# A three-stage kernel on one core: the scaling of k moved from GpSimd to VectorE, with the order around it

## The reference

```python
# 1: retention (attention with a fixed decay)
scores = q @ k.T / sqrt(D)                       # (4, 8, 576, 576)
gamma = 1 - 2.0 ** (-5 - arange(H))
Dmat = where(i >= j, gamma ** (i - j), 0)
x = (scores * Dmat) @ v                          # tokens x 512
# 2: mixture of experts: two of eight per token
noisy = x @ w_gate + log1p(exp(x @ w_noise)) * noise
two largest of noisy, softmax over the two
out[token] += weight * (relu(x[token] @ w1[e]) @ w2[e])   # 512 -> 1024 -> 512
# 3
h = out @ w_in                                   # 512 -> 2048
y = (h * cos(h)) @ w_out                         # 2048 -> 512
```

## Time and profile before

| | us |
|---|---|
| median of 3 runs | 1010.4 (1009.32 to 1011.52) |
| the profiled execution | 1012.63 |
| its span, first to last instruction | 1010.7 |

### The profile page before, as it was taken

One profiled execution on the slowest core, in us unless ns is written; L12 is line 12 of the kernel. 1 busy time (PEld: TensorE's weight loads), 2 busy tenths in 40 slices (PEclk: granted clock), 3 DMA queues, 4 the chain that ended last, 5 costly groups with the idle time before them and its releaser, 6 DMA issues.

```text
span 1010.7 us, 17316 instructions
## 1 busy us (share of the span) xinstructions
PE 982.1 (97%) x6116; PEld 887.9 (88%) x6116; DVE 482.3 (48%) x928; ACT 426.0 (42%) x779; POOL 118.2 (12%) x122
## 2 busy tenths in 40 slices
PE   8989799999999999999999989999999999999997
PEld 7878689899898989989899989999999999999996
DVE  3685464434333333333333466555555555555554
ACT  1442434333333333333334465455555555555554
POOL 4375520000000000000000131101000001010000
PEclk9996899999999999999999999999999999999999
DMA  9985552525445172544524452101010011011000
GB/s 364 308 304 208 194 202 84 197 96 177 156 129 203 62 257 75 185 147 145 187 74 148 159 192 95 42 32 42 21 52 21 21 52 37 36 34 29 31 0 32
DMA packets 64359, 122.02 MB, mean 121 GB/s; under 512 B 5696, under 2 KB 31552, under 8 KB 64320
## 3 DMA queue, kind: packets, MB, share of 16 engines
q1 hardware_dynamic: 58080, 101.05, 29.4%
q0 software_dynamic: 6240, 20.45, 6.1%
HBM read 83.73 MB, written 37.75 MB: 120 GB/s over the span
## 4 chain that ended last, share of the span: by engine, by line
PE 86%; DVE 4%; DMA 4%; issue 2%; SPq 1%; ACT 1%; another core or an unknown queue 1%; ACTq 0%; DVEq 0%
PE ps L1448 20%; PE ps L1467 20%; PE ps L1284 15%; PE ps L1302 14%; PE ps L1322 3%; PE ps L1334 3%; PE ps L1397 2%; PE ps L1409 2%; PE ps L1270 2%; DMA gath<-x_slots 2%; PE ps L1209 1%; PE ps L1240 1%; PE ps L1217 1%; DMA y_slots<-y_sb 1%; PE ps L1194 1%
## 5 line engine op out<-in xcount | busy, mean ns | idle before, releaser
L1284 PE MATMUL ps<-xs,w_hi 128*128 (+1 forms) x784 | 182.9, 312 | 0.0
L1020 DVE TENSOR_TENSOR w_lo<-raw,w_hi 128x1024 fp32r<-128x1024 f32 x48 | 58.8, 1225 | 170.0 <-ACT w_hi L665 170.0
L1284 PEld LDWEIGHTS ps<-xs,w_hi 128*128 128x128 f32 x784 | 133.1, 188 | 0.8
L1448 PE MATMUL ps<-x_hi,w_hi 128*128 (+1 forms) x384 | 130.8, 341 | 0.1
L1448 PE MATMUL ps<-x_hi,w_lo 128*128 (+1 forms) x384 | 129.1, 336 | 0.0
L1448 PE MATMUL ps<-x_lo,w_hi 128*128 (+1 forms) x384 | 129.1, 336 | 0.0
L790 ACT ACTIVATE turns<-ps 128x384 f32<-128x384 f32 x96 | 47.2, 491 | 183.7 <-PE ps L1448 183.6
L1284 PE MATMUL ps<-xs,w_lo 128*128 (+1 forms) x392 | 121.2, 309 | 0.0
L1144 DVE TENSOR_SCALAR turns<-turns 128x384 f32<-128x384 f32 x96 | 37.3, 388 | 167.6 <-ACT turns L790 167.6
L1467 PE MATMUL ps<-w_hi,g_hi 128*128 128x512 f32 x288 | 112.6, 391 | 2.1 <-DVE g_lo L1155 2.1
L1467 PE MATMUL ps<-w_hi,g_lo 128*128 128x512 f32 x288 | 113.3, 393 | 0.0
(11 more groups left out here) (169 smaller groups left out, 1674.9 us busy)
## 6 DMA issues: line engine op xcount, KB each, us to landing
raw<-weights SPq DMA_DIRECT2D x80, 512.0 KB
y_slots<-zeros_sb SPq DMA_DIRECT2D x42, 256.0 KB, 3.7
gath<-x_slots SPq DMA_DIRECT2D x40, 256.0 KB, 3.5
y_slots<-y_sb SPq DMA_DIRECT2D x40, 256.0 KB, 2.1
qk<-qk SPq DMA_DIRECT2D x18, 512.0 KB
kv<-kv SPq DMA_DIRECT2D x18, 512.0 KB, 6.2
out<-out_sb SPq DMA_DIRECT2D x18, 256.0 KB, 2.1
x_slots<-zeros_sb SPq DMA_DIRECT2D x8, 256.0 KB, 8.2
```

The lines of the kernel that those rows point to most:

```text
L1020: tt(w_lo[:, at], raw[:, f % 2, :], w_hi[:, at].bitcast(F32), ALU.subtract).then_inc(split_done, 1)
L1284: last_one = nc.tensor.matmul(ps[5 + half][:, 0:HALF], w[:, at:at + P], xs[:, bass.ds(g % 2, 1), a, k, half * HALF:(half + 1) * HALF].rear ...
L1448: last_one = nc.tensor.matmul(h_bank(f)[:, 0:TB], w[:, cols], a[:, bass.ds(par, 1), k, :].rearrange("p a s -> p (a s)"), start=k == 0 and ...
```

## The change

The scaling of k leaves GpSimd's loop and becomes `decay_k` in VectorE's. VectorE's order becomes: scale, carry, decay_k, then second choice, sums, places, first choice, split. Counts and places of the first three groups are in the same steps (8, 12, 16), the counts behind the k_dec products; that of the fourth group is issued in step 18 behind the rows. The eight zero tails are spread over steps 3 to 8 instead of 3 to 10, and chunk 4 is split at step 13 instead of 12. The two x blocks of unit 0 are transposed and their high parts copied in the last attention step (19), ahead of the last tile's logits. Unit 0 gets other PSUM banks (`x_bank`, `h_first`), a wait for `ranked` goes, the fillers are four instead of eight, and the routing of groups 3 and 4 on VectorE and the last count on TensorE are placed anew among the first products.

```diff
@@ -76,11 +76,11 @@
 SECOND_AT = {7: 0, 11: 1, 15: 2, 18: 3}
-COUNT_AT = {8: 0, 12: 1, 16: 2, 18: 3}
-PLACE_AT = {9: 0, 13: 1, 17: 2, 19: 3}
-SCATTER_AT = {10: (0,), 11: (1,), 12: (2,), 13: (3,), 14: (4,), 15: (5,), 16: (6,), 17: (7,)}
-ZERO_AT = {t: t - 3 for t in range(3, 3 + E)}
-SPLIT_AT = {4: 0, 5: 1, 8: 2, 9: 3, 12: 4, 16: 5}
+COUNT_AT = {8: 0, 12: 1, 16: 2}
+PLACE_AT = {8: 0, 12: 1, 16: 2}
+SCATTER_AT = {10: 0, 11: 1, 12: 2, 13: 3, 14: 4, 15: 5, 16: 6, 17: 7}
+ZERO_AT = {3: (0,), 4: (1,), 5: (2, 3), 6: (4, 5), 7: (6,), 8: (7,)}
+SPLIT_AT = {4: 0, 5: 1, 8: 2, 9: 3, 13: 4, 16: 5}
 LAST_ORDER = (0, 8, 9, 10, 11, 12, 13, 14, 1, 2, 3, 4, 5, 6, 7, 15)
@@ -318,7 +318,7 @@
-            return ps[j] if isinstance(g, int) and g == 0 else ps[7]
+            return ps[j if j < FRONT[0] else j + 3] if isinstance(g, int) and g == 0 else ps[7]
@@ -330,6 +330,10 @@
             return slice(0, front * BLK) if part_no == 0 else slice(front * BLK, UN)
+        def h_first(f, part_no):
+            return ps[(2, 5)[part_no] + f % 2]
@@ -415,8 +419,8 @@
                     load_chunk(SPLIT_AT[t + 1], SPLIT_AT[t + 1])
-                if t in ZERO_AT:
-                    zero_tail(ZERO_AT[t])
+                for e in ZERO_AT.get(t, ()):
+                    zero_tail(e)
             load_chunk(FE - 2, FE - 2)
@@ -528,13 +532,12 @@
-            def scatter_rows(t):
+            def scatter_rows(t, k):
                 pool.wait_ge(pos_done, group_of(t) + 1)
                 pool.wait_ge(x_done, t + 1)
-                for k in range(2):
-                    nc.gpsimd.indirect_dma_start(
-                        out=x_slots, out_offset=bass.IndirectOffsetOnAxis(ap=pos_x[:, k, t:t + 1], axis=0),
-                        in_=x_sb[t][:, :], in_offset=None).then_inc(rows_early if t < EARLY else rows_late, 16)
+                nc.gpsimd.indirect_dma_start(
+                    out=x_slots, out_offset=bass.IndirectOffsetOnAxis(ap=pos_x[:, k, t:t + 1], axis=0),
+                    in_=x_sb[t][:, :], in_offset=None).then_inc(rows_early if t < EARLY else rows_late, 16)
@@ -548,21 +551,14 @@
                                             ).then_inc(q_dec_done, 1)
-                if c < CB - 1:
-                    if t == 0:
-                        pool.wait_ge(decay_in, 16)
-                    pool.wait_ge(kv_in[t % 3], loads(t))
-                    above(pool, u_done, updates(t) - 1)
-                    kd = tab("k_decay", C)[:, c * H:(c + 1) * H].unsqueeze(2).to_broadcast((C, H, D))
-                    nc.gpsimd.tensor_tensor(k_dec[updates(t) % 2][:, :].rearrange("c (h d) -> c h d", h=H),
-                                            kv_sb[t % 3][:, 0, :].rearrange("c (h d) -> c h d", h=H),
-                                            kd, ALU.mult).then_inc(k_dec_done, 1)
                 if t == 10:
                     pool.wait_ge(x_zero, 16 * E)
-                for n in SCATTER_AT.get(t, ()):
-                    scatter_rows(n)
+                if t in SCATTER_AT:
+                    for k in range(2):
+                        scatter_rows(SCATTER_AT[t], k)
             for t in range(EARLY, NT):
-                scatter_rows(t)
+                for k in range(2):
+                    scatter_rows(t, k)
             pool.wait_ge(rows_late, 16 * 2 * (NT - EARLY))
@@ -623,6 +619,12 @@
+            def x_high(g, j):
+                act.wait_ge(tx_done, TPU * g + j + 1)
+                nc.scalar.activation(
+                    xs[:, bass.ds(g % 2, 1), 0, :, j * BLK:(j + 1) * BLK].rearrange("p a k s -> p (a k) s"),
+                    x_bank(g, j)[:, :].rearrange("p (k s) -> p k s", k=KD_TILES), ACT.Copy).then_inc(xs_hi_done, 1)
             def step(s):
@@ -635,6 +637,8 @@
                 if t == NT - 1:
+                    for j in range(FRONT[0]):
+                        x_high(0, j)
                     softplus(NG - 1)
@@ -644,12 +648,6 @@
                 step(s)
-            def x_high(g, j):
-                act.wait_ge(tx_done, TPU * g + j + 1)
-                nc.scalar.activation(
-                    xs[:, bass.ds(g % 2, 1), 0, :, j * BLK:(j + 1) * BLK].rearrange("p a k s -> p (a k) s"),
-                    x_bank(g, j)[:, :].rearrange("p (k s) -> p k s", k=KD_TILES), ACT.Copy).then_inc(xs_hi_done, 1)
@@ -677,7 +675,7 @@
                     act.wait_ge(p2_done, i - 1)
-                nc.scalar.activation(hs_hi[:, f % 2, cols], ps[5 + i % 2][:, 0:cols.stop - cols.start], ACT.Relu
+                nc.scalar.activation(hs_hi[:, f % 2, cols], h_first(f, part_no)[:, 0:cols.stop - cols.start], ACT.Relu
                                      ).then_inc(relu_done, 1)
@@ -685,8 +683,6 @@
             act.sem_inc(y_act, 3)
-            for j in range(FRONT[0]):
-                x_high(0, j)
             for f in range(FE):
@@ -917,6 +913,15 @@
+            def decay_k(t):
+                c = t % CB
+                dve.wait_ge(kv_in[t % 3], loads(t))
+                above(dve, u_done, updates(t) - 1)
+                kd = tab("k_decay", C)[:, c * H:(c + 1) * H].unsqueeze(2).to_broadcast((C, H, D))
+                nc.vector.tensor_tensor(k_dec[updates(t) % 2][:, :].rearrange("c (h d) -> c h d", h=H),
+                                        kv_sb[t % 3][:, 0, :].rearrange("c (h d) -> c h d", h=H),
+                                        kd, ALU.mult).then_inc(k_dec_done, 1)
             link(nc.vector.memset(before_sum[:, 0:E], 0.0))
@@ -924,21 +929,23 @@
             dve.wait_ge(decay_in, 16)
-            for s in range(NT + 2):
+            for s in range(NT + 1):
                 if s < NT:
                     scale(s)
+                if 0 < s <= NT and (s - 1) % CB < CB - 1:
+                    carry(s - 1)
+                if s < NT and s % CB < CB - 1:
+                    decay_k(s)
                 if s in SECOND_AT:
                     second_choice(SECOND_AT[s])
+                    sum_picks(SECOND_AT[s])
                 if s in PLACE_AT:
                     place_rows(PLACE_AT[s])
-                if 0 < s <= NT and (s - 1) % CB < CB - 1:
-                    carry(s - 1)
-                if s in SECOND_AT:
-                    sum_picks(SECOND_AT[s])
                 if s in FIRST_AT:
...
                     split_low(SPLIT_AT[s], w_hi, w_lo, SPLIT_AT[s] * CHUNK)
             def count_units():
@@ -1004,7 +1011,7 @@
                 dve.wait_ge(relu_done, i + 1)
-                stt(hs_lo[:, f % 2, cols], ps[5 + i % 2][:, 0:cols.stop - cols.start], 0.0,
+                stt(hs_lo[:, f % 2, cols], h_first(f, part_no)[:, 0:cols.stop - cols.start], 0.0,
                     hs_hi[:, f % 2, cols].bitcast(F32), ALU.max, ALU.subtract).then_inc(hs_done, 1)
@@ -1037,17 +1044,20 @@
             dve.sem_inc(y_dve, 2)
-            first_choice(NG - 1)
             for j in range(FRONT[0]):
                 x_low(0, j)
+            place_rows(NG - 2)
             h_low_first(0, 0)
+            first_choice(NG - 1)
+            h_low_first(1, 0)
             second_choice(NG - 1)
             sum_picks(NG - 1)
-            h_low_first(1, 0)
+            h_low_first(2, 0)
             place_rows(NG - 1)
...
             for f in range(2, FE):
-                h_low_first(f, 0)
+                if f > 2:
+                    h_low_first(f, 0)
                 if f == 2:
@@ -1179,6 +1189,15 @@
                 last_one.then_inc(counted, 1)
+            def transpose_x(g, j):
+                pe.wait_ge(gath_in[j], 16 * g + 16)
+                if not isinstance(g, int) or g > 0:
+                    pe.wait_ge(xs_done, TPU * g + j)
+                for k in range(KD_TILES):
+                    last_one = nc.tensor.transpose(x_bank(g, j)[:, k * BLK:(k + 1) * BLK], gath[j][:, k * P:(k + 1) * P],
+                                                   ident)
+                last_one.then_inc(tx_done, 1)
@@ -1226,7 +1245,12 @@
                         last_one.then_inc(u_done, 1)
+                if s in COUNT_AT:
+                    count(COUNT_AT[s])
                 t = s - 2
+                if t == NT - 1:
+                    for j in range(FRONT[0]):
+                        transpose_x(0, j)
                 if 0 <= t < NT:
@@ -1244,8 +1268,8 @@
                     last_one.then_inc(rows_ps_done, 1)
-                if s in COUNT_AT:
-                    count(COUNT_AT[s])
+                if t == NT - 2:
+                    count(NG - 2)
@@ -1261,15 +1285,6 @@
             pe.wait_ge(split_done, 1)
-            def transpose_x(g, j):
-                pe.wait_ge(gath_in[j], 16 * g + 16)
-                if not isinstance(g, int) or g > 0:
-                    pe.wait_ge(xs_done, TPU * g + j)
-                for k in range(KD_TILES):
-                    last_one = nc.tensor.transpose(x_bank(g, j)[:, k * BLK:(k + 1) * BLK], gath[j][:, k * P:(k + 1) * P],
-                                                   ident)
-                last_one.then_inc(tx_done, 1)
@@ -1313,14 +1328,12 @@
```

(11 more changed lines are left out.)

## The result

The kernel after the change takes 1001.02 us (median of 4 runs, 999.27 to 1001.61) where the kernel before takes 1010.71 on the same chip (4 runs, 1009.32 to 1011.52): ratio 0.9903, 95% interval [0.9886, 0.9920]. It is faster by 9.7 us, inside the range of 984 to 1003, but just under half of the 20.1 us that were forecast. The profiled execution of after took 1001.27 us, its span 999.4, against 1012.63 and 1010.7.

A forecast was written before the change was run, and what follows sets the result against it. The prediction took TensorE's waits for VectorE, the half clock behind them and the tail as the bound in the first 149 us: -13.5 - 7.5 + 0.9 = -20.1, from 1010.4 to 990.3 us, range 984 to 1003.

The forecast's parts named there:

- Attention, -13.5: Attention steps 12 to 18: TensorE's waits for VectorE and the half clock vanish, last step begins at 92.9, -13.5 us.
- The signs named for it: Attention from 61 us: scores 5.1 us apart, ret/state waits at most 0.5, full clock up to the last step, k_dec 0.6 to 1.2.
- The slack of 1 us at the mixed tile: Attention tile 13: VectorE's work behind the second places ends about 1 us before TensorE wants its bank again.
- the rival: Attention steps 8 to 17: one stall of some 3 us brings 16 us at half clock, costing 8 us: 998.3; chance 0.20.
- The tail, -7.5: Last attention step to first expert product: x tiles moved into the step, between -9.5 and -5.5 us, taken as -7.5.
- the middle: Tail: -7.5 us, taken between gains of 9.5 (scatters not the cause of the idle time) and 5.5 (they are).
- the held end: Tail: GpSimd's eight scatters cause the idle time and let go at 100.6; first expert product at 103.9, gain 5.5 us.
- the other end: Tail: scatters not the cause, TensorE's own work of 7.0 us decides; first expert product at 99.9, gain 9.5 us.
- Late rows, +0.9: Second transposes: x rows 2 to 4 wait for all scatters, the last ones 1.4 us later less 0.5 slack, +0.9 us.
- The lock follows k_dec: Attention and tail: VectorE's two-input operations still wait behind GpSimd, stalls and half clock return; 1010 or a little under; chance 0.09.
- VectorE waits for kv: Attention: kv over 3.4 us late, k_dec holds the next ret, TensorE stalls and loses clock; +19 us, 1030; chance 0.08.
- the four: Rivals: another clock fall (998.3, chance 0.20), lock stalls (1010, 0.09), late kv (1030, 0.08), larger gain (986, 0.08).

The follow-up runs named there:

- Before again: The unchanged kernel before, profiled and timed a second time, on chip 6: 1012.33 us in 8 runs, 1.0028 to its 23 other runs there.
- the later chunk load: The kernel after, with the load of weight chunk 7 issued only behind the x splits: 993.29 us on chip 3, 1001.31 on chip 6.
- the controls on chips 0 and 10: The kernel after itself, unchanged, timed beside its variants on the same chip: 1000.76 us on chip 0, 992.43 on chip 10.
- the held kernel: The kernel after, with GpSimd's late scatters held until unit 0's x tiles are split: 1004.67 us on chip 0, ratio to before 0.9952.

## Why the prediction was half right

*Attention, -13.5: right.* It came to -12.5. The missing 1.0 is a start 0.6 us later (scores of step 6 at 32.49, not 31.86) and small change. The signs named for it held: steps of 5.08 us where no count stands in them, no wait for `ret` or `state` from 30 us on, full clock up to the last step. `k_dec` took 1.06 in the mean where 0.65 + 0.45 was forecast; single ones reach 1.33, beyond the 1.2 that was named. The slack of 1 us at the mixed tile was small indeed: one execution overran it, for 5.1 us where the rival said 8. Some luck is in the number: it was read from an execution whose half clock was long. Beside the second profile of before (last step at 102.0), after on the same chip (94.0) gains 7.9 us in this piece.

*The tail, -7.5: this step failed.* It came to -2.0. "If they are not the cause ... 99.9. If they are ... 103.9. ... I take the middle". On the chip of the result the picture is that of chip 0, where the eight scatters were shown to be the cause, so the middle was 2.0 us too early to begin with (101.9 against 103.9). The first expert product came at 108.36, behind the 108 that the prediction itself had named as proof against it. The rest of the way to 108.36 is in two terms of the held end:
- "the eight scatters run from 89 to 98.9 and let go at 100.6": they ran from 90.97 to 101.44 and let go at 102.99, +2.4. The last early scatter starts at 89.70, not 88.0, ahead of them, and one of the eight took 1.63.
- "transposes 0.87 and the 2.4 of last logits, rows and fillers": 3.3 us of work took 5.4 (102.99 to 108.36), +2.1. TensorE in pieces lost its clock (0.50 from 99.1 to 109.4), as it did behind the wait of the earlier trace rows: logits 1.73 us instead of 1.06. The prediction took the scatters to hold a signal, after which all runs at full speed. In fact TensorE itself was cut to pieces, and neither that nor the half clock behind it was charged.

2.0 + 2.4 + 2.1 = 6.5, what lies between 101.9 and 108.36; 1.0 of it is the later start that was counted above, so 5.5 is the tail's own. On short-tail chips the other end held to 0.1 us: own work 7.0 forecast, 6.9 measured four times. But there before seems to have no pauses to lose either: it wasn't profiled on such a chip, but `k_dec` moved alone keeps the old tail, and that is 10.3. So -7.5 was met on neither kind: about -3.4 by this comparison on the one, -2.0 (and -1.9 on chip 6) on the other, where the pauses outlast the work that was shortened under them.

*Late rows, +0.9: +2.0.* Mis-sized by 1.1. The path was the forecast one: the last six scatters begin at 118.76 to 126.11, the last one's writes land 2.71 us later, the rows are loaded at 128.88, and TensorE waits 1.17 us for them where 0.9 was forecast. The other 0.9 us are TensorE's own: up to where the transposes could begin it took 22.2 us instead of 21.6, the first products being still at half clock, and the eight transposes 1.31 instead of 1.03. The end of the chain:

```profile
124.84 0.96 POOL x_slots L538
125.80 0.30 issue
126.11 2.71 DMA x_slots<-x_sb,pos_x
128.88 2.77 DMA gath<-x_slots
131.70 1.31 PE ps L1198 x8
```

*Untouched stages.* +2.0 in stage 3, which the prediction left out, and -0.9 in the units. Before again took 423.0 from stage 3's start where its first profile took 421.6, and the kernels built on after took 421.6 to 423.9: single executions differ by that much, and it can't be put down to the change.

*The start of the count.* The forecast took 20.1, read from an execution 2.2 us above the median, off the median itself. Profile to profile the gain is 11.4, between medians 9.7: 1.7 us of the -20.1 belonged to that execution, most likely to its long half clock. With this the account closes: 1.0 (attention) + 5.5 (tail) + 1.1 (late rows) + 2.0 (stage 3) - 0.9 (units) + 1.7 = 10.4, the 20.1 forecast less the 9.7 measured. That the time still fell inside the range is owed to its width.

*The rivals.* "The lock follows k_dec": the lock is there, without a price for TensorE. "VectorE waits for kv": no such wait is on the path. The case that came is none of the four: it is the worse end of the tail's own range, and then 3.4 us beyond it (14.4 where that end gave 11.0), by the pauses and the clock.

No kernel tried is below after: the later chunk load is within its noise, the others lose.

## What to carry to other kernels

When a profile shows time that nothing explains ("unknown", "issue", "remote") and it lies over one other engine's run of instructions, make that run the first suspect, and move it by one wait to see whether the time goes along; here it did. As long as it is there, shortening the work under it buys little (2.0 us here). Don't take the middle between "it is the cause" and "it is not": give each case its price and its chance, and add the half clock that TensorE may pay after the stall (6.8 to 17.1 us at 0.50 in these traces). And a gain read from a stalled execution has to be counted from that execution's time, then set against the median's.

## What the chip showed beyond the question

- A row of indirect scatters from GpSimd (0.96 us each, 0.30 between) can disturb TensorE, on some chips. 3 to 9 us into the row its products start 0.7 us apart, and its signals reach other engines up to 11 us late (products done at 106.06, `hs_hi` at 117.21 on chip 0). In the worst case such a signal comes back to TensorE as a stop of 7.0 us. Chips 0 and 6 and that of the result showed it (14.4 to 15.8 us of tail in after and its variants), chips 3, 8 and 10 did not (6.9). The traffic was about the same on both kinds: 363 and 383 GB/s from 96 to 101 us in the controls on chips 0 and 10, a DMA share of 0.54 and 0.53 from 105 to 110 us in the held kernel, 0.54 and 0.43 from 110 to 115. The control on chip 10 moved the more and wasn't disturbed, so the amount alone doesn't make the difference. What does, and what TensorE and the scatters share, stays open. The Trainium skill (SBUF — State Buffer, section "Who interferes with whom") has it that a DMA never contends with a compute engine. The tails of 6.9 us on chips 3, 8 and 10 agree; on chip 0 TensorE was held up beside the scatters, and there the measurement decides.
- The kernel before is itself 3 to 7 us slower on those chips (1009.1 to 1010.7 against 1003.5 to 1006.0), so the ratios lie close together (0.9903, 0.9907, 0.9913 against 0.9857 and 0.9898) while the stages behind them differ.
- A VectorE operation of 128x32 and two SBUF inputs took up to 2.98 us beside GpSimd's pair of 128x512 (`t_c`, usual 0.18), and 1.25 beside a single one.
